# Order of the Nyquist row and of two weight splits in an attention, gated-MLP and Fourier kernel on one core

## The chip, the cores and the metric

The kernel runs on one NeuronCore of a Trainium2 chip. Its engines are called here as in the profile: PE (TensorE, matrix products; PEld is its weight load), DVE (VectorE), ACT (ScalarE), POOL (GpSimd) and SP (SyncE, which only issues DMAs). Each engine runs its own list of instructions in order, and engines wait for each other on semaphores. The metric is the device time of one execution in microseconds (us), and less is better. The time before is the median of three runs: 718.55, 721.84 and 721.86, so 721.84 us.

## The reference, cut to what matters

Three stages follow each other, for 4 batches (B) of 768 tokens (S) with 8 heads of 48 channels, 384 in all. The changes lie in the third stage and in the loading of its first weight.

```python
def _attn_ref(q, k, v, alpha):            # decayed linear attention
    for t in range(S):
        state = alpha[:, :, t, :, None] * state + np.einsum('bhd,bhe->bhde', k[:, :, t], v[:, :, t])
        y[:, :, t] = np.einsum('bhd,bhde->bhe', q[:, :, t], state)

def _moe_ref(x, w_in, g_ln, w_sg, b_sg, w_out):
    h = gelu_tanh(x @ w_in)
    u, v = (h[..., :d_ff // 2], h[..., d_ff // 2:])
    v_n = (v - mu) / np.sqrt(var + 1e-06) * g_ln
    v_s = np.einsum('ts,bsd->btd', w_sg, v_n) + b_sg[None, :, None]
    return x + (u * v_s) @ w_out

def _moe2_ref(x, w_ch1, w_ch2):
    X = np.fft.fft(np.fft.fft(x, axis=1), axis=2)
    u = x + np.real(X)
    un = (u - mu) / np.sqrt(var + 1e-06)
    return u + np.maximum(un @ w_ch1, 0.0) @ w_ch2
```

## The kernel before

*Numbers.* Large products run on float32r operands that are split into a hi part and a lo part; each product is three passes (hi x hi, hi x lo, lo x hi), `product`, L1178. Weights come from DRAM in pieces of 128 x 1536 (768 KB). Pieces 0 to 5 are `w_in`, `w_out`, `w_sg`; 6 to 8 are w_c1 (`w_ch1`; in rows `w_c`, or `w_c_0_117`, `w_c_1_118` for the first two); 9 to 11 are `w_c2`. A piece is split in one of two ways. The usual way: SP loads the raw piece into a stage, ACT copies it with a cast (hi, `split_hi`, L739), and DVE subtracts (lo = raw - hi, `split_lo`, L895). The other, for the pieces in `SUMMED` = (2, 3, 4): ACT writes -hi into the lo tile (`negative`, L744), and POOL issues a DMA that adds the raw piece from DRAM onto it (`sum_lo`, L693). `load_piece` decides when a stage is free: once the lo part of the piece before in the same stage is there, or, for a piece in `SUMMED`, its hi part. `wait_lo` is the consumer's wait.

*Stages of the work.* Phase 1 of batch b does the gated MLP of batch b and the attention of batch b + 1 beside it. Its steps stand in a table: "v" and "u" are the products with `w_in`, "s" 0 to 7 are the eight products with `w_sg`. After the product of s i PE does the `w_out` product of i - 1, which reads `gated_lo`. For every s DVE makes `gated` in two operations (L1025, L1029), ACT its hi part (L802), DVE its lo part (L971). In s 4 DVE also makes `x_half` (`add_x`, L979) from the banks that PE writes next. Phase 2 of batch b does the MLP with w_c1 ("h") and w_c2 ("o") and, beside it, the Fourier steps of batch b + 1. The Fourier steps of batch 0 stand beside phase 1 of the last batch, where there is no attention left to do (`LAST_P1_AT`). Phase 2 of batches 1 and 2 is one loop, run twice, on PE, ACT and DVE; phase 2 of batch 0 is code of its own. So the mixes of batch 0 run in the last phase 1, of batch 1 in phase 2 of batch 0, of batches 2 and 3 in the first and second pass of the loop. POOL and SP run without a loop.

*Fourier steps*, in the function `mixing` of each engine, in the order of `P2_AT`, `P2_FIRST_AT` and `LAST_P1_AT`:
- "fold", "folded": DVE adds mirrored quarters of the tokens (`x_quarters`; half of them are loaded by SP, the mirrored half by four indirect DMAs of POOL, L660), then hi and lo parts.
- "z": PE products with `seq_dft` into `FB[i % 3]` (FB are banks 5 to 7), and ACT copies them to `z` (L815).
- "nyquist": PE makes one row of output, the middle token (L1376, 2 instructions, 4 records of 97 columns), in columns 0 to 193 of `FB[1]`; ACT copies it (L818).
- "mix": PE makes all three tiles at once (L1388, 24 instructions, 48 records), tile i into `FB[TB[i]]`, `TB` = (2, 0, 1), so the third tile overwrites the row's bank and first waits for ACT's copy (`ahr_done`). ACT copies tile i (`even_odd`, L822), DVE makes sum and difference (L1072, L1073) and adds them to the residual rows (`u_new`, L1079, L1080), for i = 0 also the Nyquist row (L1086, L1087). The residual rows are loaded by `load_residual` on SP (L564, L567) and on POOL (three indirect DMAs, L660).
- "stats": DVE mean and variance; "norm", "turn", "turned": normalization, transposition, hi and lo parts of `ut`, the input of phase 2.

What sets the order: the tables at the top of the file, one for all engines, and each engine picks its part of a step. POOL's part of "mix" i is not run at "mix" in the last phase 1 but at "stats" i; in phase 2 it is run at "mix" i (`mixing` of POOL, L684 and L687, which waits for `mv2_done` of that tile's statistics). POOL issues the mirrored quarters of batch b + 2 where its list has "nyquist", ahead of its own part of that step.

SP's list at the place in question is: raw load of piece 6, raw load of piece 7 (same stage, so it waits for piece 6), the residual rows of batch 0, the store of x1, raw load of piece 8.

## Time and profile before

| what | value |
|---|---|
| time, median of three runs | 721.84 us |
| the three runs | 718.55, 721.84, 721.86 us |
| profiled execution: time, span | 720.12 us, 718.3 us |
| granted PE clock, mean | 0.995 |
| PE busy | 701.0 us, 98% |
| DVE busy | 451.8 us, 63% |
| ACT busy | 198.4 us, 28% |
| POOL busy | 80.0 us, 11% |

The span is the time from the first to the last instruction of the profiled execution. Busy time counts an engine's own operations; waits and DMA issues are not in it. PE busy is close to the whole span, and records of matmuls overlap each other, since they are pipelined.

### The profile page before, as it was taken

The page shows a single profiled execution, that of the slowest core. Times are in us where ns is not written, and L with a number is a line of the kernel's source. Part 1 is how long each engine was busy: PE and PEld are TensorE (multiplying, and loading weights), DVE is VectorE, ACT ScalarE, POOL GpSimd, SP SyncE. Part 2 cuts the span into 40 slices and gives each one's busy share as a digit, 9 for nine tenths or more (in the row PEclk, how much of TensorE's full clock was granted, in tenths as well). Part 3 has the DMA queues.
Part 4 walks back from the last instruction along what each step waited for, and adds up shares of the span by engine and source line. Part 5 has one row for each costly group of instructions (what it writes and reads, how often), then busy time and mean ns, then how long its engine had stood idle before and what let it go on. Part 6 is the DMA issues. An engine that isn't in the chain of part 4 may idle for free.

```text
span 718.3 us, 13452 instructions
## 1 busy us (share of the span) xinstructions
PE 701.0 (98%) x5578; PEld 670.6 (93%) x5578; DVE 451.8 (63%) x869; ACT 198.4 (28%) x369; POOL 80.0 (11%) x124
## 2 busy tenths in 40 slices
PE   7799989999999999999999999999999999999998
PEld 6689989889998999989999999999999999999998
DVE  7997868897768977668687747372543817331212
ACT  1438111242113411134415332232211422222111
POOL 1023000030001200042110512002210101000000
PEclk9999999999999999999999999999999999999999
DMA  9757132231332223061324403002110200000000
GB/s 295 208 139 182 52 100 84 83 97 55 91 93 71 63 54 97 35 212 44 112 77 165 144 20 92 1 34 67 53 59 1 76 23 33 0 34 1 5 29 34
DMA packets 21214, 55.90 MB, mean 78 GB/s; under 512 B 2388, under 2 KB 14808, under 8 KB 21160
## 3 DMA queue, kind: packets, MB, share of 16 engines
q1 hardware_dynamic: 18104, 44.53, 20.1%
q0 software_dynamic: 2912, 10.47, 5.6%
q8 instruction: 40, 0.66, 0.4%
q10 hardware_dynamic: 144, 0.13, 0.1%
q14 instruction: 14, 0.11, 0.1%
HBM read 45.66 MB, written 9.46 MB: 77 GB/s over the span
## 4 chain that ended last, share of the span: by engine, by line
PE 86%; DVE 10%; issue 2%; ACT 1%; DMA 1%; DVEq 0%; SPq 0%
PE bank L1178 74%; PE bank L1209 3%; PE bank L1241 2%; PE bank L1236 1%; PE bank L1273 1%; PE bank L1402 1%; PE bank L1388 1%; PE bank L1226 1%; DVE fwd L927 1%; DVE rev L915 1%; PE bank L1199 1%; DVE u_kept L1138 1%; DMA decay_k_q<-in_akq 1%; DVE sm L945 1%; DVE gated L1029 1%
## 5 line engine op out<-in xcount | busy, mean ns | idle before, releaser
L1178 PE MATMUL bank<-ut_hi,w_c 128*128 128x384 f32 x576 | 162.6, 338 | 0.0
L1125 DVE SCALAR_TENSOR_TENSOR hidden_lo<-bank,hidden_hi 128x384 fp32r<-128x384 f32 x96 | 53.3, 556 | 155.5 <-ACT hidden_hi L849 154.9
L1178 PEld LDWEIGHTS bank<-ut_hi,w_c 128*128 128x128 f32 x576 | 105.4, 188 | 0.4
L849 ACT ACTIVATE hidden_hi<-bank 128x384 fp32r<-128x384 f32 x96 | 47.2, 492 | 201.6 <-PE bank L1178 200.5
L1178 PE MATMUL bank<-w_c_hi,hidden_hi 128*128 128x384 f32 x288 | 96.6, 335 | 0.5 <-DVE u_kept L1138 0.5
L1178 PE MATMUL bank<-ut_lo,w_c 128*128 128x384 f32 x288 | 96.3, 334 | 0.0
L1178 PE MATMUL bank<-w_c_hi,hidden_lo 128*128 128x384 f32 x288 | 96.3, 334 | 0.0
L1178 PE MATMUL bank<-w_c_lo,hidden_hi 128*128 128x384 f32 x288 | 96.2, 334 | 0.0
L1178 PE MATMUL bank<-w_sg_hi,vn_hi 128*128 128x384 f32 x192 | 67.1, 350 | 0.0
L1178 PE MATMUL bank<-w_sg_lo,vn_hi 128*128 128x384 f32 x192 | 64.9, 338 | 0.0
L1178 PE MATMUL bank<-w_sg_hi,vn_lo 128*128 128x384 f32 x192 | 64.9, 338 | 0.0
L802 ACT CAST gated_hi<-gated 128x384 fp32r<-128x384 f32 x32 | 16.4, 513 | 152.2 <-DVE gated L1029 152.2
L1178 PEld LDWEIGHTS bank<-w_c_hi,hidden_hi 128*128 128x128 f32 x288 | 54.1, 188 | 1.5 <-issue 1.4
L1178 PEld LDWEIGHTS bank<-ut_lo,w_c 128*128 128x128 f32 x288 | 54.2, 188 | 0.0
L1178 PEld LDWEIGHTS bank<-w_c_lo,hidden_hi 128*128 128x128 f32 x288 | 54.1, 188 | 0.0
L1178 PEld LDWEIGHTS bank<-w_c_hi,hidden_lo 128*128 128x128 f32 x288 | 54.1, 188 | 0.0
L1178 PEld LDWEIGHTS bank<-w_sg_hi,vn_hi 128*128 128x128 f32 x192 | 36.5, 190 | 1.9
L1178 PEld LDWEIGHTS bank<-w_sg_hi,vn_lo 128*128 128x128 f32 x192 | 36.6, 191 | 0.0
L1178 PEld LDWEIGHTS bank<-w_sg_lo,vn_hi 128*128 128x128 f32 x192 | 36.5, 190 | 0.0
L1178 PE MATMUL bank<-w_out_hi,gated_hi 128*128 128x384 f32 x96 | 32.7, 340 | 2.0 <-DVE x_half L979 1.4
L1178 PE MATMUL bank<-x_hi,w_in_hi 128*128 128x384 f32 x96 | 32.9, 342 | 0.0
L945 DVE TENSOR_TENSOR sm<-bank,constants 128x512 f32<-128x512 f32 x42 | 27.0, 684 | 8.5 <-PE bank L1209 8.4
(193 smaller groups left out, 1339.8 us busy)
## 6 DMA issues: line engine op xcount, KB each, us to landing
decay_k_q<-in_akq SPq DMA_DIRECT2D x19, 673.8 KB, 5.0
x_scratch<-x_half SPq DMA_DIRECT2D x8, 579.0 KB
out_tiles<-u_kept SPq DMA_DIRECT2D x24, 192.0 KB, 2.0
values<-in_v SPq DMA_DIRECT2D x18, 192.0 KB, 5.0
x_quarters<-x_scratch SPq DMA_DIRECT2D x16, 168.9 KB
raw_first_a<-in_w_first SPq DMA_DIRECT2D x3, 768.0 KB, 10.2
raw_first_b<-in_w_first SPq DMA_DIRECT2D x3, 768.0 KB
raw_weights_b<-in_w_second SPq DMA_DIRECT2D x3, 768.0 KB
```

What stands on the lines that cost most here:

```text
L802: nc.scalar.copy(gs[0][:, i % 3, :], gt[:, i % 3, :]).then_inc(ghi_done, 1)
L849: nc.scalar.activation(hid[0][:, i % 4, :], HB[i % 2][:, 0:HS], ACT.Relu).then_inc(hhi_done, 1)
L915: nc.vector.tensor_tensor_scan(rev[:, NA - 2::-1], raw[:, NA - 1:0:-1], resets[:, NA - 1:0:-1], 1.0, ALU.mult, ALU.add).then_inc(rev_done, 1)
L927: nc.vector.tensor_tensor_scan(fwd[:], raw[:, 0:NA], resets[:], 0.0, ALU.mult, ALU.add).then_inc(fwd_done, 1)
L945: nc.vector.tensor_tensor(sm[:, :, x, :], sc[x][:].rearrange("p (a t) -> p a t", a=4), mask[:].unsqueeze(1).to_broadcast([P, 4, P]), ALU.m ...
L1029: nc.vector.tensor_tensor(gt[:, i % 3, :], gt[:, i % 3, :], ug[:, f, h * HS:(h + 1) * HS], ALU.mult).then_inc(gt_done, 1)
L1125: nc.vector.scalar_tensor_tensor(out=hid[1][:, i % 4, :], in0=HB[i % 2][:, 0:HS], scalar=0.0, in1=f32(hid[0][:, i % 4, :]), op0=ALU.max, o ...
L1138: nc.vector.tensor_tensor(ub[:, HT * i + j, :], ACC[j][:, 0:DM], ub[:, HT * i + j, :], ALU.add).then_inc(fin_done, 1)
L1178: ins = nc.tensor.matmul(dst, a, c, start=start and n == 0, stop=stop and n == len(passes) - 1)
L1199: ins = nc.tensor.transpose(ky[:, g * PR:(g + 1) * PR], kd[:, g, :], ident[0:PR, 0:PR])
L1209: ins = nc.tensor.matmul(sc[j][:, g * P:(g + 1) * P], kd[at, g, :], qu[at, g, :], start=True, stop=True)
L1241: ins = nc.tensor.matmul(ky[q, h * D:(h + 1) * D], sm[:, g, j, q], values[:, h * D:(h + 1) * D], start=c == 0, stop=True, skip_group_check ...
```

## The change

Four things are changed.

1. Table order: in `P2_AT`, `P2_FIRST_AT` and `LAST_P1_AT` the step "nyquist" follows "mix" 0, where it stood ahead of it.
2. The Nyquist row is no longer in columns 0 to 193 of `FB[1]` but in the free columns behind the mix tiles: its even half in `FB[0]`, its odd half in `FB[1]`, columns 388 to 484 of each. PE's wait for the row's copy in the middle of the mixes goes. ACT copies the row in two instructions; its copies of mix tiles 1 and 2 also wait for the row's product.
3. Pieces 6 and 7 (the first two of w_c1) join `SUMMED`: DVE's subtraction goes, ACT gets a negation each, and POOL a DMA each that adds onto SBUF. The stage that pieces 6, 7 and 8 share is then free once the hi part is made.
4. In `LAST_P1_AT` ACT's hi copy of piece 6 stands behind the four z steps, where it stood ahead of them, and that of piece 7 behind the second mix, where it stood ahead of the first. The negation follows each, and POOL's `sum_lo` stands at the same place.

```diff
-SUMMED = (2, 3, 4)
+SUMMED = (2, 3, 4, 6, 7)
...
-         10: [("nyquist", 0), ("mix", 0)], 11: [("stats", 0)], 12: [("mix", 1)], 13: [("stats", 1)], 14: [("mix", 2)], 15: [("stats", 2)],
+         10: [("mix", 0), ("nyquist", 0)], 11: [("stats", 0)], 12: [("mix", 1)], 13: [("stats", 1)], 14: [("mix", 2)], 15: [("stats", 2)],
...
-              ("s", 1): [("split", 6), ("z", 0), ("z", 1), ("z", 2), ("z", 3)],
-              ("s", 2): [("nyquist", 0), ("split", 7), ("mix", 0), ("stats", 0)],
-              ("s", 3): [("mix", 1), ("stats", 1)], ("s", 4): [("mix", 2)],
+              ("s", 1): [("z", 0), ("z", 1), ("z", 2), ("z", 3), ("split hi", 6), ("neg", 6)],
+              ("s", 2): [("mix", 0), ("nyquist", 0), ("stats", 0)],
+              ("s", 3): [("mix", 1), ("stats", 1), ("split hi", 7), ("neg", 7)], ("s", 4): [("mix", 2)],
...
+            def sum_lo(n):
+
+                pool.wait_ge(w_neg_done, SUMMED.index(n) + 1)
+                src, m = (w_first, n) if n < NP1 else (w_second, n - NP1)
+                pool.dma_start(pieces[n][1], src[:, m * PIECE:(m + 1) * PIECE],
+                               accum_op=ALU.add).then_inc(w_sum_in[n], 16)
...
+                            if what == "neg":
+                                sum_lo(n)
...
                 if step == "nyquist":
                     act.wait_ge(ny_done, m + 1)
-                    nc.scalar.copy(by_channel(fourier_tiles(m)[4][:]), by_parity(FB[1][0:1, 0:NL])).then_inc(ahr_done, 1)
+                    for odd in range(2):
+                        ins = nc.scalar.copy(by_channel(fourier_tiles(m)[4][:])[:, 0, odd], FB[odd][0:1, 2 * NL:2 * NL + KQ])
+                    ins.then_inc(ahr_done, 1)
                 if step == "mix":
                     act.wait_ge(mix_done, 2 * (KD * m + i + 1))
+                    if i > 0:
+                        act.wait_ge(ny_done, m + 1)
...
                 if step == "nyquist":
-                    pe.wait_ge(z_kept, 4 * m + 2)
                     for odd in range(2):
-                        ins = nc.tensor.matmul(FB[1][0:2, odd * KQ:(odd + 1) * KQ], zz[0:KQ - odd, 0, odd, HS:HS + 2],
+                        ins = nc.tensor.matmul(FB[odd][0:2, 2 * NL:2 * NL + KQ], zz[0:KQ - odd, 0, odd, HS:HS + 2],
                                                cs[0:KQ - odd, 0, odd, :], start=True, stop=True)
                     ins.then_inc(ny_done, 1)
                 if step == "mix" and i == 0:
                     pe.wait_ge(z_kept, 4 * (m + 1))
                     for i, e in itertools.product(range(HT), range(2)):
-                        if i == 2 and e == 0:
-                            pe.wait_ge(ahr_done, m + 1)
```

ACT's list in the last phase 1, before the change, from the `gated` of step s 1 to the second mix tile:

```order
L802 CAST gated_hi<-gated 128x384
L739 CAST w_c_0_117<-raw_weights_b 128x1536
L815 COPY z<-bank 97x2x194
L815 COPY z<-bank 96x2x194
L815 COPY z<-bank 97x2x194
L815 COPY z<-bank 96x2x194
L802 CAST gated_hi<-gated 128x384
L818 COPY nyquist_row_early<-bank 1x2x97
L739 CAST w_c_1_118<-raw_weights_b 128x1536
L822 COPY even_odd_early<-bank 128x2x2x97
L802 CAST gated_hi<-gated 128x384
L822 COPY even_odd_early<-bank 128x2x2x97
```

The same stretch of ACT's list after the change (`w_c_0_117<-w_c_0_117` is the negation):

```order
L807 CAST gated_hi<-gated 128x384
L820 COPY z<-bank 97x2x194
L820 COPY z<-bank 96x2x194
L820 COPY z<-bank 97x2x194
L820 COPY z<-bank 96x2x194
L744 CAST w_c_0_117<-raw_weights_b 128x1536
L749 ACTIVATE w_c_0_117<-w_c_0_117 128x1536
L807 CAST gated_hi<-gated 128x384
L831 COPY even_odd_early<-bank 128x2x2x97
L824 COPY nyquist_row_early<-bank 1x97 x2
L807 CAST gated_hi<-gated 128x384
L831 COPY even_odd_early<-bank 128x2x2x97
```

The hi copy of piece 6 has moved behind the z copies, with its negation. The hi copy of piece 7 has left this stretch; it comes right after its last row. SP's list has the same rows in the same order as before.

POOL's list from the x1 columns of the last phase 1 (`x_half`) to the second variance step of batch 1, before the change (`ve`, `rs` are the variance step):

```order
L651 COPY x_half<-x_half 128x3x2
L660 DMA x_quarters<-x_scratch,mirrored_rows 112x386 x4
L660 DMA u_new<-x_scratch,mirrored_rows 128x386 x3
L660 DMA x_quarters<-x_scratch,mirrored_rows 112x386 x4
L684 TENSOR_TENSOR ve_61<-mv_59,eps_c 128x2
L687 TENSOR_TENSOR rs_60<-ve_61,minus_half 128x2
L684 TENSOR_TENSOR ve_61<-mv_59,eps_c 128x2
L687 TENSOR_TENSOR rs_60<-ve_61,minus_half 128x2
```

The same stretch after the change:

```order
L658 COPY x_half<-x_half 128x3x2
L669 DMA x_quarters<-x_scratch,mirrored_rows 112x386 x4
L669 DMA u_new<-x_scratch,mirrored_rows 128x386 x3
L693 TENSOR_TENSOR ve_61<-mv_59,eps_c 128x2
L696 TENSOR_TENSOR rs_60<-ve_61,minus_half 128x2
L669 DMA x_quarters<-x_scratch,mirrored_rows 112x386 x4
L693 TENSOR_TENSOR ve_61<-mv_59,eps_c 128x2
L696 TENSOR_TENSOR rs_60<-ve_61,minus_half 128x2
```

The second group of four quarter loads (those of batch 2, beside the mixes of batch 1) has moved behind the first variance step. The same happens once more, a batch later.

## Rows read from the trace of the kernel before

**Rows 1.** The page: busy us (share) of PE to POOL; the chain by engine.
```profile
PE 701.0 (98%) x5578; PEld 670.6 (93%) x5578; DVE 451.8 (63%) x869; ACT 198.4 (28%) x369; POOL 80.0 (11%) x124
PE 86%; DVE 10%; issue 2%; ACT 1%; DMA 1%; DVEq 0%; SPq 0%
```

**Rows 2.** Waits of PE: who waited for whom, us in total, times, longest.
```profile
PE bank L1178 <- DVE x_half L979: 1.4, 1, 1.4
...
PE bank L1388 <- issue: 0.7, 2, 0.4
```

**Rows 3.** Timeline of PE, last phase 1: start, us, instruction, [idle before, releaser].
```profile
363.51 0.33 PE L1178 MATMUL bank<-w_out_hi,gated_hi 128*128 128x384 f32 x1
...
369.76 0.41 PE L1178 MATMUL bank<-w_out_hi,gated_hi 128*128 128x384 f32 x1 [1.41 <-DVE x_half L979]
```

**Rows 4.** Timeline of DVE, last phase 1.
```profile
351.53 0.62 DVE L1025 SCALAR_TENSOR_TENSOR gated<-bank,g_col,bias_sg 128x384 f32<-128x384 f32 x1 [3.88 <-PE bank L1178]
...
355.25 1.76 DVE L895 TENSOR_TENSOR w_c<-raw_weights_b,w_c 128x1536 fp32r<-128x1536 f32 x1 [1.37 <-ACT w_c L739]
...
357.68 0.56 DVE L1079 TENSOR_TENSOR u_new_early<-u_new_early,sum_diff_early 128x386 f32<-128x386 f32 x1
...
362.38 0.56 DVE L971 TENSOR_TENSOR gated_lo<-gated,gated_hi 128x384 fp32r<-128x384 f32 x1 [0.58 <-ACT gated_hi L802]
...
368.13 1.48 DVE L979 TENSOR_TENSOR x_half<-bank,y_by_token_odd 128x384 f32<-128x384 f32 x3
```

**Rows 5.** Timeline of PE at the mixes of batches 0, 1 and 3.
```profile
353.41 2.24 PE L1388 MATMUL bank<-chan_dft,z 97*64 97x97 f32 x48
...
430.48 1.98 PE L1388 MATMUL bank<-chan_dft,z 97*64 97x97 f32 x41
432.83 0.56 PE L1388 MATMUL bank<-chan_dft,z 96*64 96x97 f32 x7 [0.36 <-issue]
...
591.04 0.50 PE L1376 MATMUL bank<-chan_dft,z 97*2 97x97 f32 x4
591.47 2.24 PE L1388 MATMUL bank<-chan_dft,z 97*64 97x97 f32 x48
```

**Rows 6.** Timeline of ACT: last z copy, piece 7, first mix copies of batches 1, 3.
```profile
348.38 0.50 ACT L815 COPY z<-bank 96x388 f32<-96x388 f32 x1 [0.59 <-PE bank L1178]
...
353.75 1.46 ACT L739 CAST w_c<-raw_weights_b 128x1536 fp32r<-128x1536 f32 x1
...
432.94 0.51 ACT L822 COPY even_odd<-bank 128x388 f32<-128x388 f32 x1 [2.01 <-PE bank L1388]
...
592.44 0.52 ACT L822 COPY even_odd<-bank 128x388 f32<-128x388 f32 x1 [0.53 <-PE bank L1388]
```

**Rows 7.** Timeline of POOL beside the mixes of batch 1.
```profile
430.95 0.92 POOL L660 DMA_INDIRECT x_quarters<-x_scratch,mirrored_rows  x1 [0.30 <-issue]
437.82 0.18 POOL L684 TENSOR_TENSOR ve<-mv,eps_c 128x2 f32<-128x2 f32 x1 [5.94 <-DVE mv L1099]
...
443.90 0.22 POOL L684 TENSOR_TENSOR ve<-mv,eps_c 128x2 f32<-128x2 f32 x1 [5.10 <-DVE mv L1099]
```

**Rows 8.** Timeline of SP's DMA issues: piece 7 and the residual of batch 0.
```profile
347.67 0.36 SPq L515 DMA_DIRECT2D raw_weights_b<-in_w_second  x1
348.38 0.38 SPq L564 DMA_DIRECT2D u_new_early<-x_scratch  x1
```

**Rows 9.** DMA queues, 353 to 354 us, then 41 to 42: packets, MB, engines' share.
```profile
q0 software_dynamic: 124, 0.39, 101.7%
q1 hardware_dynamic: 5, 0.00, 1.3%
...
q0 software_dynamic: 33, 0.20, 98.9%
q1 hardware_dynamic: 2, 0.01, 3.1%
```

**Rows 10.** DMA issues by tile: KB each, median us from issue to landing.
```profile
w_out_lo<-in_w_first POOLq DMA_DIRECT2D x1, 768.0 KB, 8.0
```

More of the change, by code:

```diff
@@ L118 @@
                6: [("fold", 0)], 7: [("fold", 1)], 8: [("fold", 2), ("fold", 4)], 9: [("fold", 3), ("folded", 0)],
-               10: [("fold", 5), ("folded", 1), ("z", 0)], 11: [("z", 1), ("z", 2)], 12: [("z", 3)], 13: [("nyquist", 0), ("mix", 0)],
+               10: [("fold", 5), ("folded", 1), ("z", 0)], 11: [("z", 1), ("z", 2)], 12: [("z", 3)], 13: [("mix", 0), ("nyquist", 0)],
                14: [("stats", 0)], 15: [("mix", 1)], 16: [("stats", 1), ("mix", 2)], 17: [("stats", 2)],
@@ L688, in mixing @@
                                             ALU.pow).then_inc(rs2_done, 1)
-            def sum_lo(n):
-                pool.wait_ge(w_neg_done, SUMMED.index(n) + 1)
-                pool.dma_start(pieces[n][1], w_first[:, n * PIECE:(n + 1) * PIECE],
-                               accum_op=ALU.add).then_inc(w_sum_in[n], 16)
             for step, t in FIRST_POOL:
@@ L731, in beside_last_phase1 @@
                         split_hi(n)
+                    elif what == "neg":
+                        negative(n)
                     elif what in FOURIER_STEPS:
@@ L1422, in phase2 @@
                             pe.wait_ge(sb_done, 8 * B)
-                            wait_lo(pe, NP1 + KD - 2)
+                            for n in range(NP1, NP1 + KD - 1):
+                                wait_lo(pe, n)
                             product(HB[0][:, 0:HS], terms[:KD - 1], stop=False)
```

## The prediction

> **What bounds the kernel now.** I read the busy shares and the chain of waits first, then who waited on TensorE (PE), then the timelines around each of those waits, and last the DMA windows. PE is busy 98% of the span of 718.3 us and is 86% of the chain that ended last [rows 1]. So only two things can move the time: fewer PE instructions, or the few gaps in which PE stands. The change takes no matmul away (below), so the gaps are the whole prize. Within its reach are two kinds [rows 2]: one wait of 1.4 us for `x_half`, and "issue" gaps in front of mix matmuls, two times.
>
> The first [rows 3]: PE waits 1.41 us for VectorE's (DVE) `x_half` addition before it may start the `w_out` product at 369.76. The DVE timeline [rows 4] says why that is late. DVE idles 1.37 us until ScalarE (ACT) has made the hi copy of the second w_c1 piece, subtracts for 1.76 us from 355.25, and starts its first mix addition at 357.68; from there on work is queued one behind the other up to `x_half` at 368.13 to 369.61. Whatever DVE gains before 357.68 arrives at `x_half`, until PE's 1.41 us are used up.
>
> The second [rows 5]: a mix group has 48 matmul records. In batches 0 and 3 they run through in 2.24 us. In batch 1 there are 41, a hole, and 7 more, from 430.48 to 433.39: 2.91 us, so 0.67 us lost. Batch 2 reads the same, and the wait list counts two such gaps. ACT sees the first mix tile late too: its `even_odd` copy starts at 432.94, 2.46 us after the group's first record, against 592.44 - 591.47 = 0.97 us in batch 3 [rows 5, 6]. What batches 1 and 2 share, and 0 and 3 don't, is that GpSimd (POOL) is issuing the mirrored quarters of the following batch just then; in batch 1 its fourth indirect DMA runs from 430.95 to 431.87 [rows 7]. That is a coincidence of rows, not a proof.
>
> **The change part by part.**
>
> (a) Nyquist row behind the mixes. PE: four matmul records per batch stay four, now last instead of first. In batch 3 they take 591.47 - 591.04 = 0.43 us [rows 5], paid either way. The step from 384-column products to small ones is at one end of the group before and at the other now; nothing in the rows tells its cost apart, so I take 0, and as bounds a third of those 0.43 us in each of four places either way, 0.6 us. The wait for the row's copy in the middle of the mixes goes; in batch 3 the group ran through with it, so it held nobody: 0. ACT: one copy becomes two of 97 columns. The nearest row is the even_odd copy, 0.51 us for 388 columns [rows 6]; two copies cost at most 1.0 us and at least half of one, 0.25, in place of one that lies between. ACT is idle for 2 us before such steps [rows 6], so 0. DVE's row additions need these copies. The row is ready on PE some 2.7 us after the group's start (2.24 + 0.43) and copied by 3.5. DVE has the first tile at 0.97 + 0.51, and spends four operations, some 1.9 us, on it: 3.4. So 0.1 us on an engine that has slack there.
>
> (b) What moves with it on POOL. The order shows it: the four indirect `x_quarters` DMAs hang on the step "nyquist", POOL's variance step on "mix", and these two have changed places. POOL now waits for the statistics of the first mix, computes, and only then issues. In batch 1 the variance step starts at 437.82 [rows 7] and takes about 1 us, so the DMAs go out from 438.8 on, no longer at 427. They take 1.24 us each, to 443.8, and the next variance step stood at 443.90 in before [rows 7]: it fits with nothing to spare, and what comes after it (the normalization) waits for a third one anyway. The quarters are read by the folds of the next batch, tens of us later. Queued behind the waiting POOL instruction is nothing else. So the move costs 0, and the mixes of batches 1 and 2 lose their neighbour. I take the rows at their word: these mixes then look like batch 3's, -0.67 us twice, -1.34. Bounds: 0 (another cause) and -1.34.
>
> The Trainium skill, "Runtime: NRT & Kernel Launch", Instruction fetch mechanics, says that prefetch of instructions is sequential, in blocks, and that a taken branch breaks it. Batch 3 is the second pass of a loop whose first pass is batch 2, so a fetch stall would part them too, and (b) would bring nothing. Batch 0 is run for the first time as well and has no hole [rows 5], which speaks against it.
>
> (c) lo parts of the first two w_c1 pieces by accumulating DMA. DVE loses two subtractions of 1.76 us. The first lies before an idle time of 3.88 us [rows 4]: 0. The second stands in the queue above. With it gone, and ACT's hi copy (1.46 us from 353.75 [rows 6]) no longer ahead of the even_odd copy, that copy runs 0.97 us after the group's start, which is 353.41 - 0.43, so at 353.95, and DVE is through its two differences by 355.2: 2.5 us ahead of 357.68. ACT gains two negations; the nearest row is its hi copy of the same size, 1.46 us [rows 6]. The first pair (hi copy, negation) starts when the z copies end at 348.88 and ends at 351.8; the next thing ACT has to do comes with DVE's `gated` of 351.53 + 1.2 [rows 4]. The second pair lies behind the second mix copy, about 361.5 to 364.5; the `gated` of s4 is not there before 364.7. Cost 0, and one of 0.5 us if all comes early.
>
> But what is late next? DVE's first mix addition needs the residual rows, and the change delays their loading. On SP's queue the load of w_c1 piece 7 stands ahead of the residual. In before they went out at 347.67 and 348.38 [rows 8]. Now the hi copy of piece 6 stands behind four z copies (last ends 348.88 [rows 6]) and ends at 350.36, and only then does SP go on: 2.7 us later. In before SP's queue had moved all but 5 packets of both by 353 [rows 9]; 2.7 later is 355.7. POOL's three indirect residual loads, which keep their time, ran behind SP's in before (q0 with 101.7% of the engines' time from 353 to 354 [rows 9]) and now are ahead of them or between: they moved 0.6 MB at 0.39 MB in a us, 1.5 us. Of that 0 to 1.5 falls on SP's loads; I take 1.0. With 0.5 us until the semaphore is seen DVE starts at 357.2 instead of 357.68: -0.48 us. Lower end 356.2 (nothing ahead), the full -1.41. Upper end: the accumulating DMA of piece 6, issued at 352.5 behind POOL's indirects. One like it landed 8.0 us after its issue [rows 10], here 360.5; if it goes ahead, the residual is there at 361.3, +3.6 us. I take 357.2 since the engines serve first what came first: from 41 to 42 us an accumulating transfer on q0 has 98.9% of their time, and the SP load asked for 1.4 us after it 3.1% [rows 9].
>
> The Trainium skill, "DMA: Bandwidth & Descriptors", Queues, rings and completion order, says instead that an engine takes turns between queues packet by packet. By it the residual would share with the accumulating transfer from about 354 on and be there near 359, +1.3 us.
>
> Nobody waits for the two sums: the second is issued near 366 and lands near 374, and PE reads these pieces in phase 2, after 384. Their 1.5 MB may put off the load of piece 8 by 2 us; it has 11 us until ACT wants it.
>
> **Sum.** Against the profiled execution (span 718.3, whole time 720.12): -0.48 - 1.34 = -1.8, span 716.5. The three runs of before are 718.55, 721.84 and 721.86, so its profile lies between them. From the median: 721.84 - 1.8 = 720.0 us.
>
> **Rivals.**
> 1. *The residual comes late (slower).* Place: DVE before its first mix addition, waiting for SP's residual load. Every us beyond 357.68 arrives at PE, first in front of `w_out` of s3 (slack 363.51 - 362.94 = 0.57 us [rows 3, 4]), the rest at `x_half`. It decides from 359.0 on, where it has eaten the 1.34 us. With a landing at 360.2, between an even sharing and the upper end, it is +2.5 - 1.34 = +1.2: 723.0 us. For it: an accumulating transfer holds the engines fully at 0.20 MB in a us, half the rate of the others [rows 9]. Against: the residual is asked for 1.6 us before it.
> 2. *The holes at the mixes stay*, POOL's DMAs not being their cause: -0.5, so 721.4 us. For it: POOL's data also moves during batch 0's mixes (353 to 354 [rows 9]), and no hole comes. Against: the four batches split exactly as POOL's issuing does.
> 3. *Everything comes.* The residual is there by 356.3: -1.41 - 1.34 = -2.8, so 719.1 us. POOL's loads would have to be nearly through by 351; in before nothing of them had moved by then.
>
> **How the numbers follow.** Forecast 40%, rival 1 22%, rival 2 25%, rival 3 13%. A measurement of this kernel doesn't tell less than about 0.5% (3.6 us); its own runs lie 3.3 us apart. All cases lie within that, and only scatter or the far ends bring the time out of it. Faster by over 0.5% (below 718.2): half of rival 3 and a sixth of the forecast, 0.13. Slower (above 725.4): a third of rival 1, 0.07. Same: 0.80. Range 717.8 to 723.6: it takes in all four cases with some scatter, and leaves out the upper end of rival 1 and the lowest medians.
>
> **What the new profile would show.** Right: mixes of batches 1 and 2 without a hole, and `even_odd` about 1.0 us after their first record in all; POOL's quarters near 439; PE's wait for `x_half` near 0.9 us; DVE's wait before its first mix addition ended by a DMA, near 357. Wrong: holes of 0.7 us still there (rival 2); a wait of PE for `gated_lo` of s3, or a longer one for `x_half` (rival 1). A new gap on PE of over 1 us elsewhere, behind POOL's moved DMAs or at the start of phase 2, would break what I called hidden.

## The result: 723.35 us, slower than before by 0.36%

Timed side by side, the changed kernel takes 723.35 us (median of 22 runs, 718.99 to 726.37) and the kernel before 720.17 us (22 runs, 717.95 to 721.86). The ratio is 1.0036, with a 95% interval of 1.0022 to 1.0049: 1.6 to 3.5 us more. The forecast was 1.8 us less. The time lies inside the range and within the 0.5% called "same", but it moved to the other side: what happened is rival 1, at more than its price. That it lies inside the range is in part luck: the forecast started from 721.84 us, the median of three runs, and the median of 22 is 1.7 us lower. The loss of 3.2 us is larger than the 1.8 us that the range allowed above its start.

**The profile after.** The profiled execution has a span of 724.6 us and takes 726.37 us, the slowest of its 22 runs. It is 6.3 us longer than the profiled execution of before, and 2.5 us of that lie ahead of the changed place: the mixes of batch 0 begin at 355.45, where they began at 352.98. There PE's clock was low for longer after gaps near 101 to 103 us (granted 0.57 on average from 102 to 110, before 0.79). What follows is therefore read behind the start of these mixes. The page, as in [rows 1]:

```profile
PE 702.5 (97%) x5578; PEld 672.6 (93%) x5578; DVE 448.1 (62%) x867; ACT 201.8 (28%) x375; POOL 82.5 (11%) x126
PE 82%; DVE 10%; DMA 4%; issue 2%; ACT 1%; SPq 0%; DVEq 0%
```

PE has the same 5578 matmul records, and DMA has grown from 1% to 4% of the chain that ended last. PE's waits, against [rows 2] (us in total, times, longest):

```profile
PE bank L1187 <- DVE gated_lo L980: 4.6, 3, 4.1
```

The wait for `x_half` and the two gaps with "issue" in front of mix matmuls are gone from the list. In their place stands one wait of 4.1 us for `gated_lo`. PE's timeline around it, the counterpart of [rows 3, 5] (start, us, instruction, [idle before, releaser]):

```profile
355.45 2.24 PE L1394 MATMUL bank<-chan_dft,z 97*64 97x97 f32 x48
357.63 0.50 PE L1384 MATMUL bank<-chan_dft,z 97*2 97x97 f32 x4
...
365.79 0.34 PE L1187 MATMUL bank<-w_sg_hi,vn_lo 128*128 128x384 f32 x1
370.27 0.69 PE L1187 MATMUL bank<-w_out_hi,gated_hi 128*128 128x384 f32 x1 [4.14 <-DVE gated_lo L980]
370.75 0.52 PE L1187 MATMUL bank<-w_out_lo,gated_hi 128*128 128x384 f32 x1
371.07 0.52 PE L1187 MATMUL bank<-w_out_hi,gated_lo 128*128 128x384 f32 x1
...
375.77 0.33 PE L1187 MATMUL bank<-w_sg_hi,vn_lo 128*128 128x384 f32 x1
375.95 0.33 PE L1187 MATMUL bank<-w_sg_hi,vn_hi 128*128 128x384 f32 x1
...
437.69 2.24 PE L1394 MATMUL bank<-chan_dft,z 97*64 97x97 f32 x48
```

Two things are to be seen besides the gap. The mixes of batch 1 run through in 2.24 us, without the hole (those of batch 2 and 3 too, from 512.60 and 597.32). And behind the gap the starts of neighbouring matmuls lie 0.32 us apart until 375.5, and 0.17 or 0.18 from 375.77 on. The stretches say why (us; busy us and count of PE, PEld, DVE, ACT, POOL; granted clock of PE; DMA share, GB/s):

```profile
360.00:364.00 4.00, 4.00 (x25) 4.00 (x24) 0.00 (x0) 0.00 (x0) 0.00 (x0) 1.00 0.90 182
366.00:368.00 2.00, 0.13 (x1) 0.00 (x0) 1.89 (x8) 0.00 (x0) 0.00 (x0) 1.00 0.00 0
368.00:370.00 2.00, 0.00 (x0) 0.00 (x0) 1.39 (x3) 0.89 (x3) 0.91 (x2) 0.70 0.00 0
371.00:372.00 1.00, 1.00 (x4) 1.00 (x4) 0.96 (x3) 0.97 (x2) 0.00 (x0) 0.50 0.00 0
374.00:375.00 1.00, 1.00 (x5) 1.00 (x4) 0.42 (x2) 0.61 (x2) 1.00 (x2) 0.50 0.00 0
376.00:378.00 2.00, 2.00 (x13) 2.00 (x12) 1.87 (x5) 0.00 (x0) 0.24 (x1) 1.00 0.92 141
```

PE stood for 4.1 us, and the granted clock fell to 0.50 (1.2 of 2.4 GHz) in the gap and came back only near 375.6. So the gap costs twice: the 17 steps from 370.27 to 375.77 take 5.50 us, and at the full clock's 0.173 us each they would take 2.95, another 2.55 us.

The first line of that table holds the cause: from 360 to 364 DVE and ACT do nothing at all. DVE's timeline, against [rows 4]:

```profile
356.98 0.36 DVE L1081 TENSOR_TENSOR sum_diff_early<-even_odd_early 128x194 f32<-128x194 f32 x1 [0.63 <-ACT even_odd_early L831]
...
364.97 0.56 DVE L1088 TENSOR_TENSOR u_new_early<-u_new_early,sum_diff_early 128x386 f32<-128x386 f32 x1 [7.36 <-DMA x_middle_row_early<-x_scratch]
...
369.65 0.56 DVE L980 TENSOR_TENSOR gated_lo<-gated,gated_hi 128x384 fp32r<-128x384 f32 x1 [0.58 <-ACT gated_hi L807]
```

DVE has the difference of the first mix tile early, as meant, and then waits 7.36 us for the last of the residual rows, the 1.5 KB middle row. Counted from the first record of PE's mix group, the first mix addition starts at 364.97 - 355.45 = 9.52 us; before it was 357.68 - 352.98 = 4.70 [rows 4], and PE's row there is 0.43 us ahead of the mixes. SP issues that load here (against [rows 8]):

```profile
353.15 0.43 SPq L564 DMA_DIRECT2D u_new_early<-x_scratch  x1
353.62 0.39 SPq L567 DMA_DIRECT2D x_middle_row_early<-x_scratch  x1
```

and POOL its accumulating transfer of piece 6 another 1.1 us later:

```profile
353.76 0.95 POOL L669 DMA_INDIRECT u_new_early<-x_scratch,mirrored_rows  x1 [0.30 <-issue]
354.71 1.02 POOL L648 DMA_DIRECT2D w_c<-in_w_second  x1
```

The DMA queues in the windows 358 to 359, 359 to 360, 360 to 361 and 361 to 362 (packets, MB, share of 16 engines), q1 being SP's and q0 POOL's:

```profile
q1 hardware_dynamic: 144, 0.22, 70.7%
q0 software_dynamic: 23, 0.10, 39.2%
...
q0 software_dynamic: 53, 0.18, 88.0%
q1 hardware_dynamic: 54, 0.07, 22.0%
...
q0 software_dynamic: 33, 0.19, 98.0%
q1 hardware_dynamic: 8, 0.01, 2.8%
...
q0 software_dynamic: 35, 0.22, 105.4%
q1 hardware_dynamic: 3, 0.00, 1.5%
```

The trace's records of single packets show three steps. Ahead of the residual on SP's own queue is the raw load of piece 7, 128 packets of 6144 bytes that begin from 353.80 to 357.98. The residual and the middle row are 385 packets of 1536 bytes from 356.74 on, and 370 of them have begun by 360. The accumulating transfer, issued at 354.71 behind POOL's own residual loads, begins its first packet at 359.30, so it meets only the tail. The last 15 packets come in at 1 to 5 in a us (the 8 of q1 above hold three of 4 bytes), with 1 to 3% of the engines, while the accumulating transfer has 96 to 105% from 360 to 363. The tail has two strings of packets. One is at 361.11, 361.64, 362.17 and 362.70. This is the end of the other, each packet of which takes 0.079 us:

```
start us   362.22   362.76   363.29   363.82   364.36
```

They are 0.53 us apart. The packets of q0 (6144 bytes) take 0.479 us each (median of its 128). The records don't name the DMA engine, but the spacing fits one small packet behind each big slow one on the two engines that still have rows to move. The last lands at 364.43, and DVE starts 0.54 us later.

**Where the time went.** From the first record of a mix group to that of the next batch's, before and after: batch 0 to 1 77.08 and 82.24 us, +5.16; batch 1 to 2 75.60 and 74.91, -0.69; batch 2 to 3 85.38 and 84.72, -0.66. The first is 4.14 for the gap, 2.55 for the clock and -1.41 for the `x_half` wait that is gone, 5.3 in all. The sum is +3.8; the medians say +3.2. The seven runs with a mean granted clock of 0.990 or 0.991 have a median of 724.3 us, the seven with 0.995 one of 721.8. That fits runs that lose less to the clock at this gap, but it isn't shown: only the profiled run has a clock by place, and part of its low clock lies near 103 us.

### The profile page after: what moved, and what is told of

Read it like the earlier page. It is cut to its first block, busy times and chain, and to the rows that moved or that the text cites. A ratio compares the mean times of both kernels' runs of the same rounds, so it can differ in the third digit from the quotient of the medians.

```text
span 724.6 us, 13457 instructions
## 1 busy us (share of the span) xinstructions
PE 702.5 (97%) x5578; PEld 672.6 (93%) x5578; DVE 448.1 (62%) x867; ACT 201.8 (28%) x375; POOL 82.5 (11%) x126
## 3 DMA queue, kind: packets, MB, share of 16 engines
HBM read 47.23 MB, written 9.46 MB: 78 GB/s over the span
## 4 chain that ended last, share of the span: by engine, by line
PE 82%; DVE 10%; DMA 4%; issue 2%; ACT 1%; SPq 0%; DVEq 0%
PE bank L1187 72%; PE bank L1218 3%; PE bank L1250 2%; DMA x_middle_row_early<-x_scratch 2%; PE bank L1245 1%; DMA w_sg_lo<-in_w_first 1%; DMA decay_k_q_b<-in_akq 1%; DVE rev L924 1%; PE bank L1408 1%; PE bank L1282 1%; PE bank L1394 1%; DVE fwd L936 1%; PE bank L1208 1%; PE bank L1235 1%; DVE u_kept L1147 1%
```

## The experiments

Each ratio is against the kernel before, timed on the same chip beside it. The twelve profiled executions differ by up to 3.5 us already ahead of the changed place (batch 0's mixes begin between 351.91 and 355.45 us), so I read each trace also by a stretch: from the first record of batch 0's mix group to the end of the span. "Start" is when DVE begins its first mix addition, counted from that same record.

| kernel | median, us | before, us | ratio (95%) | stretch, us | start, us |
|---|---|---|---|---|---|
| before | | 720.17 | | 365.3 | 4.70 |
| after | 723.35 | 720.17 | 1.0036 (1.0022 to 1.0049) | 369.15 | 9.52 |
| nyq_only | 718.1 | 720.95 | 0.9956 (0.9942 to 0.997) | 363.9 | 4.14 |
| sums_only | 725.2 | 720.95 | 1.0058 (1.004 to 1.0076) | 369.95 | 9.46 |
| residual_first | 719.03 | 720.95 | 0.9975 (0.9964 to 0.9987) | 363.5 | 4.24 |
| sum_late | 719.8 | 720.95 | 0.9984 (0.9973 to 0.9995) | 364.0 | 4.72 |
| plain_six (one run) | 721.67 | 719.35 | | 367.2 | 6.41 |
| pool_moved | 718.96 | 719.35 | 0.9996 (0.9981 to 1.0012) | 363.9 | |
| pool_back | 722.04 | 719.35 | 1.0056 (1.0032 to 1.008) | 368.3 | 9.01 |
| seven_only | 717.73 | 719.35 | 0.9973 (0.9958 to 0.9987) | 363.0 | 2.29 |
| nyq_again | 718.49 | 719.74 | 0.9984 (0.9971 to 0.9997) | 363.4 | 4.14 |
| seven_again | 718.35 | 719.74 | 0.9978 (0.9964 to 0.9993) | 362.8 | 2.36 |

### The two halves of the change: nyq_only, sums_only

nyq_only has the Nyquist row behind the mixes and what moves with it on POOL, and leaves the weights as before:

```diff
-SUMMED = (2, 3, 4, 6, 7)
+SUMMED = (2, 3, 4)
-              ("s", 1): [("z", 0), ("z", 1), ("z", 2), ("z", 3), ("split hi", 6), ("neg", 6)],
-              ("s", 2): [("mix", 0), ("nyquist", 0), ("stats", 0)],
-              ("s", 3): [("mix", 1), ("stats", 1), ("split hi", 7), ("neg", 7)], ("s", 4): [("mix", 2)],
+              ("s", 1): [("split", 6), ("z", 0), ("z", 1), ("z", 2), ("z", 3)],
+              ("s", 2): [("split", 7), ("mix", 0), ("nyquist", 0), ("stats", 0)],
+              ("s", 3): [("mix", 1), ("stats", 1)], ("s", 4): [("mix", 2)],
```

> The Nyquist part alone (row behind the mixes, free columns, POOL's quarters behind the first variance step); weights split as before. Theory (the two parts add up, and the loss sits in the weights part): no hole in any of the four mix groups, PE wait for x_half stays near 1.4 us, time 1.3 us below before (ratio 0.998). Rival (the loss comes from the Nyquist part, from POOL's moved DMAs): a new gap in phase 2 or slower than before.

sums_only is the other half: the weights of after, with the row's old banks, waits and order in all tables. In the last phase 1:

```diff
-              ("s", 2): [("mix", 0), ("nyquist", 0), ("stats", 0)],
+              ("s", 2): [("nyquist", 0), ("mix", 0), ("stats", 0)],
```

> The accumulating transfers for pieces 6 and 7 alone, Nyquist row and its order as before. Theory: DVE waits some 7 us for the residual, PE waits 4 us for gated_lo and then has the clock at 0.5 for 5 us, and the two holes of 0.67 us at the mixes stay: 5.2 us above before (ratio 1.007), the slowest of the four. Rival (noise or the Nyquist part makes the loss): within 1 us of before.

Measured: one half is faster than before, the other slower, by its stretch and its median ratio by more than the whole change, though the two intervals overlap. PE of sums_only, then of nyq_only:

```profile
367.81 0.44 PE L1183 MATMUL bank<-w_out_hi,gated_hi 128*128 128x384 f32 x1 [4.07 <-DVE gated_lo L976]
...
435.28 2.06 PE L1393 MATMUL bank<-chan_dft,z 97*64 97x97 f32 x42
437.64 0.55 PE L1393 MATMUL bank<-chan_dft,z 96*64 96x97 f32 x6 [0.30 <-issue]
```
```profile
430.69 2.24 PE L1394 MATMUL bank<-chan_dft,z 97*64 97x97 f32 x48
```

sums_only has the 4.1 us gap and keeps the holes at the mixes of batches 1 and 2. In nyq_only all mixes run through (`x48` in 2.24 us), and PE's wait for `x_half` is 0.86 us. So the loss is the weights' and the gain the Nyquist half's: by the stretch +4.6 and -1.4. These don't add up to the +3.85 of after exactly (+3.2). The clock is a part of that. Behind its gap of 4.07 us sums_only had the full clock again from 372 on, 4.2 us after PE resumed, and lost 1.7 us by the starts of its matmuls; after had it 5.4 us after PE resumed and lost 2.55. So gaps of nearly the same length didn't cost the same.

### What makes the residual late: residual_first, sum_late, plain_six

residual_first is after with two lines of SP's list exchanged:

```diff
-            load_piece(sp, NP1 + 1)
             load_residual(0)
+            load_piece(sp, NP1 + 1)
```

> The changed kernel with SP's residual load ahead of the raw load of piece 7. Theory A (the loss is the delay on SP's queue, which puts the residual's tail beside the accumulating transfer): the residual lands before 356 us on before's scale, DVE does not wait for it, PE has no wait for x_half: 2.7 us below before (ratio 0.996). Theory B (the accumulating transfer would slow the residual wherever it stands): DVE still waits some us and the time is at or above before.

sum_late is after with POOL's accumulating transfer of piece 6 put behind the first tile's statistics, so that it can't run beside the residual's loads:

```diff
-                            if what == "neg":
+                            if (what, n) == ("neg", 7):
                                 sum_lo(n)
                             if what == "stats":
                                 mixing(0, "mix", n)
+                                if n == 0:
+                                    sum_lo(6)
```

> The changed kernel with POOL's accumulating DMA of piece 6 behind the first statistics step instead of right behind the residual loads; SP's queue stays as in the changed kernel. Theory A (the delay on SP's queue alone makes the loss): DVE's wait stays several us, as long as in the changed kernel. Theory B (the accumulating transfer beside the residual makes it): DVE starts its first mix addition near my forecast's time, some 4 us after the first record of the mix group, PE's gap shrinks below 1.4 us, and the time is 1.8 us below before (ratio 0.9975).

plain_six is after with piece 6's transfer on POOL as a plain copy of the same bytes at the same place; it leaves out the addition.

```diff
-                pool.dma_start(pieces[n][1], src[:, m * PIECE:(m + 1) * PIECE],
-                               accum_op=ALU.add).then_inc(w_sum_in[n], 16)
+                if n == 6:
+                    pool.dma_start(pieces[n][1], src[:, m * PIECE:(m + 1) * PIECE].bitcast(F32R)).then_inc(w_sum_in[n], 16)
+                else:
+                    pool.dma_start(pieces[n][1], src[:, m * PIECE:(m + 1) * PIECE],
+                                   accum_op=ALU.add).then_inc(w_sum_in[n], 16)
```

> The changed kernel with POOL's DMA of piece 6 as a plain copy of the same bytes to the same tile at the same place in its queue: it leaves out the addition, so the lo part of piece 6 is the raw piece. Theory C (the accumulation makes the transfer hold the engines twice as long, and with that it starves SP's queue): DVE's first mix addition comes near 5 us after the first record of the mix group, against 9.5 in the changed kernel, and PE's gap is under 1 us. Rival (any 768 KB on POOL's queue there does it): DVE's wait is within 1 us of the changed kernel's 7.4.

DVE's first mix addition in residual_first, in sum_late and in plain_six:

```profile
358.03 0.56 DVE L1088 TENSOR_TENSOR u_new_early<-u_new_early,sum_diff_early 128x386 f32<-128x386 f32 x1 [2.09 <-DMA u_new_early<-x_scratch,mirrored_rows]
```
```profile
358.94 0.56 DVE L1090 TENSOR_TENSOR u_new_early<-u_new_early,sum_diff_early 128x386 f32<-128x386 f32 x1 [2.57 <-DMA x_middle_row_early<-x_scratch]
```
```profile
359.10 0.56 DVE L1091 TENSOR_TENSOR u_new_early<-u_new_early,sum_diff_early 128x386 f32<-128x386 f32 x1 [4.26 <-DMA x_middle_row_early<-x_scratch]
```

Either remedy alone takes the loss away; both kernels are faster than before. In residual_first SP's rows have landed at 352.58, 1.2 us ahead of the mix group, and they are no longer the last: DVE now waits 2.09 us for POOL's mirrored rows, a wait I had not listed. Those rows share the engines with the raw load of piece 7 from 352.5 on, and from 355.8 on with the accumulating transfer behind them. PE still waits 0.96 us for `x_half`, so this kernel falls short of the 2.7 us expected of it. In sum_late SP's issue is as late as in after (2.31 us ahead of the mix group, there 2.30, before 4.60), and no accumulating transfer is in its way. The last row lands 4.29 us after the group's first record, and the addition starts at 4.72, the same as before. PE's wait for `x_half` is still 1.45 us. So the later issue eats the gain and no more. With a plain transfer beside it the start is 6.41, with the accumulating one 9.52: 1.7 us for sharing the engines at all, and 3.1 us more with the slow packets. These are single traces; other kernels with the accumulating transfer in this place have 9.46 (sums_only) and 9.01 (pool_back). In plain_six the last small packets of one string of q1 are 0.30 to 0.33 us apart (357.08, 357.38, 357.68, 357.99, 358.31), beside q0's packets of 0.26 us (median of 128): the same taking of turns, at a shorter beat. The queue of the plain transfer from 357 to 358:

```profile
q0 software_dynamic: 67, 0.39, 104.0%
```

PE's gaps there are 1.04 us for `gated_lo` and 1.81 us for `x_half`.

### What made the holes at the mixes: pool_moved, pool_back

pool_moved is the kernel before with only POOL's quarter loads put behind the variance step:

```diff
-                    if (step, i) == ("nyquist", 0) and b + 2 < B:
-                        load_quarters(b + 2)
                     mixing(b + 1, step, i)
+                    if (step, i) == ("mix", 0) and b + 2 < B:
+                        load_quarters(b + 2)
```

> The kernel before with one thing changed: POOL issues the quarters of the following batch behind its first variance step, as in the changed kernel; the Nyquist row stays ahead of the mixes, with PE's wait for its copy in their middle. Theory P (POOL's DMAs beside the mixes make the holes): no hole in batches 1 and 2, 1.3 us below before (ratio 0.998). Rival Q (PE's wait for the row's copy inside the group makes them): both holes of 0.67 us stay, time as before.

pool_back is after with these loads at their old time, ahead of the variance step:

```diff
-                    if (step, i) == ("nyquist", 0) and b + 2 < B:
+                    if (step, i) == ("mix", 0) and b + 2 < B:
```

> The changed kernel with one thing undone: POOL issues the quarters of the following batch ahead of its first variance step, beside the mixes, as before. Theory P: holes of about 0.7 us are back in batches 1 and 2 and the time is 1.3 us above the changed kernel's (ratio to before near 1.006). Rival Q: no holes, the time as the changed kernel's (1.0036).

PE of pool_moved at batch 1, then POOL and PE of pool_back:

```profile
430.52 2.24 PE L1388 MATMUL bank<-chan_dft,z 97*64 97x97 f32 x48
```
```profile
433.01 0.93 POOL L669 DMA_INDIRECT x_quarters<-x_scratch,mirrored_rows  x1 [0.30 <-issue]
434.24 0.93 POOL L669 DMA_INDIRECT x_quarters<-x_scratch,mirrored_rows  x1 [0.30 <-issue]
```
```profile
433.34 2.24 PE L1394 MATMUL bank<-chan_dft,z 97*64 97x97 f32 x48
```

ACT beside the same groups: the row's copy in before, then the first mix copy in pool_moved and in pool_back:

```profile
430.59 0.34 ACT L818 COPY nyquist_row<-bank 1x194 f32<-1x194 f32 x1 [1.50 <-issue]
```
```profile
431.49 0.52 ACT L822 COPY even_odd<-bank 128x388 f32<-128x388 f32 x1 [0.53 <-PE bank L1388]
```
```profile
434.31 0.54 ACT L831 COPY even_odd<-bank 128x388 f32<-128x388 f32 x1 [1.93 <-PE bank L1394]
```

Moving POOL's loads alone closes the holes, and its stretch is 1.4 us shorter, the forecast's 1.34. But in pool_back they are issued right beside the mixes, and, against what I expected, there is no hole either. ACT's first mix copy follows the group's first mix record by 0.97 us in both, where with a hole it took 2.46 [rows 5, 6]. So POOL's loads are one condition of a hole and not its whole cause: the other is something of the old group, its order or the wait for the row's copy in its middle, or the timing, since POOL's last load begins 0.47 us after the first mix record in before and 0.90 us after it in pool_back. The wait alone didn't hold PE: in before the copy that it is for ended at 430.93, and the hole opens at 432.46, 41 records in, where the third tile begins with the 33rd. Moving POOL's loads and the new place of the row each remove the holes alone, and the gain is had once. The medians of pool_moved, 0.4 us apart, don't show the 1.4 us; the interval (-1.4 to +0.9 us) just touches it. A kernel meant to part the order of the row from the wait in the middle (row_first_free: the row ahead of the mixes in the free columns, without the wait) gave no time, so how the conditions work together stays open.

### The version without the loss: seven_only, nyq_again, seven_again

Piece 6 is split in the usual way, ahead of the z steps; only piece 7 is by the accumulating transfer, late in phase 1.

```diff
-SUMMED = (2, 3, 4, 6, 7)
+SUMMED = (2, 3, 4, 7)
-              ("s", 1): [("z", 0), ("z", 1), ("z", 2), ("z", 3), ("split hi", 6), ("neg", 6)],
+              ("s", 1): [("split", 6), ("z", 0), ("z", 1), ("z", 2), ("z", 3)],
```

> The changed kernel with piece 6 split in the usual way ahead of the z copies and only piece 7 by the accumulating DMA, so that SP goes on as early as in before and no accumulating transfer runs beside the residual. Theory: DVE does not wait for the residual and is 1.8 us ahead at the first mix addition, PE waits neither for x_half nor for gated_lo for more than 0.3 us; 2.8 us below before (ratio 0.996) and at or below the kernel with the Nyquist part alone. Rival (accumulating transfers in this stretch cost wherever they are, by the x1 store and the load of piece 8 behind them): at or above the Nyquist part alone (0.9956) by over 1 us.

Both seven_only and nyq_only had come out faster than before, but not side by side, so the two were timed again beside each other, on another chip.

> The Nyquist part alone once more, beside the version with piece 7 alone: by the traces from the start of batch 0's mixes to the end it took 363.9 us, before 365.3, so 1.4 us below before (ratio 0.998). If the 3.2 us measured earlier are real and not scatter of the first 350 us, the ratio comes at 0.9956 again.

> Piece 7 alone by the accumulating DMA, with the Nyquist part, on the same chip as the Nyquist part alone: by the traces 363.0 against 363.9 us from batch 0's mixes on, so 0.9 us faster than the Nyquist part alone (ratio to before 0.9968 against 0.998). If the accumulating transfer of piece 7 cost as much as it frees, the two would be equal within 0.2 us in that stretch.

Side by side they are 0.14 us apart in the median, which these runs can't tell from nothing. Each is faster than before by an interval that leaves out 1, and after was slower than before. The 0.9 us that I expected between them isn't shown, nor were the 2.8 us below before expected of seven_only (1.6 measured, 2.3 by the stretch). nyq_only's first ratio of 0.9956 (5 runs, another chip) did not come again: its second is 0.9984. The two traces still differ by what the weights' half was meant to bring. DVE of nyq_again, then of seven_again:

```profile
355.04 1.76 DVE L904 TENSOR_TENSOR w_c<-raw_weights_b,w_c 128x1536 fp32r<-128x1536 f32 x1 [0.81 <-ACT w_c L744]
...
357.47 0.56 DVE L1088 TENSOR_TENSOR u_new_early<-u_new_early,sum_diff_early 128x386 f32<-128x386 f32 x1
```
```profile
356.89 0.56 DVE L1088 TENSOR_TENSOR u_new_early<-u_new_early,sum_diff_early 128x386 f32<-128x386 f32 x1 [0.21 <-DMA u_new_early<-x_scratch,mirrored_rows]
```

The subtraction is gone, the addition starts 1.8 us sooner after the group's start (2.36 against 4.14), and the wait of PE for `x_half`, 0.8 us in nyq_again's list, doesn't occur in seven_again's. The stretches are 363.4 and 362.8.

## Why the prediction was wrong

**The failed step** is the residual's term of part (c): "I take 357.2 since the engines serve first what came first". It was worth -0.48 us in the sum. Measured, the addition started 4.8 us later than before, counted from the group's start, and the term with all that hangs on it came to +5.2 us. The forecast had all rows landed at 356.7, which is 3.7 us after the group's start. In sum_late, without the accumulating transfer beside them, they landed at 4.3; in after at 9.0. So the delay of SP's issue and POOL's own loads were sized 0.6 us too low, which is what the -0.48 us hung on, and the accumulating transfer, which the forecast put at nothing, is the other 4.7. The 0.5 us from landing to DVE's start was right (0.54). Three pieces make up the difference.

1. *The order of service.* The rows I rested on [rows 9] show an accumulating transfer with 98.9% of the engines and a later load with 3.1%. I read this as "the first has the engines". It shows as well what becomes of any load beside such a transfer, first or not: two small packets got in. In after the load was asked for 1.1 us earlier than the transfer, got its bulk through by 360, and its tail was slowed to one packet per 0.53 us. The Trainium skill, "DMA: Bandwidth & Descriptors", Queues, rings and completion order, has the rule: every engine goes round the queues that have work for it, a packet at a time. The trace agrees on the turns, with 0.53 us between small packets beside big ones of 0.479. It differs on their size: the page gives a packet typically 9 to 17 descriptors, and here single records of 1536 bytes took turns with single records of 6144. My estimate by that rule, +1.3 us, was too low since it shared the time evenly between queues; packets of 1536 and 6144 bytes, at 0.079 and 0.479 us, share it 1 to 6.
2. *The upper end was too low.* Even with all in its way I had the addition at 361.3, 8.3 us after the group's start. It came at 9.52.
3. *The clock.* No term stood for what a gap of PE does to PE's clock. In the trace of before the longest gap at this place was 1.41 us [rows 3], and no loss behind it was to be seen. Behind 4.14 us it was 2.55 us more. Elsewhere in the trace of before the clock did fall behind a shorter gap: PE waited 1.53 us ahead of 101.79 and was busy 0.47 of the 2 us from 100 to 102, and the granted clock averages 0.52 from 103 to 106.

**Rival 1 is what happened**, by its mechanism and at its place: PE waits first for `gated_lo` of s 3. Its price, +1.2 us, was for a landing 7.2 us after the group's start and without the clock. The gap itself follows from its own rule: 4.82 us later, less the slack of 0.57, is 4.25; it was 4.14.

**The sign that I named held**: "a wait of PE for `gated_lo` of s3 (rival 1)".

**The holes (part b)**: -1.34 forecast, -0.69 and -0.66 measured. The size and the remedy were right, and pool_moved shows that the move is enough. The reason is only half right: I took what parts batches 1 and 2 from 0 and 3 for the cause, and pool_back shows that a second condition is needed. Against it I had set the rule on fetching instructions (the Trainium skill, "Runtime: NRT & Kernel Launch", Instruction fetch mechanics), which ties a stall to a taken branch. The trace doesn't bear it out: the loop's jump back lies ahead of batch 3, which has no hole, and pool_moved, whose PE list is that of before, has none in batch 2 either.

**POOL's move at no cost**: right in effect. The loads go out from 445.78 on, behind the variance step:

```profile
444.61 0.19 POOL L693 TENSOR_TENSOR ve<-mv,eps_c 128x2 f32<-128x2 f32 x1 [30.69 <-DVE mv L1108]
...
445.78 0.99 POOL L669 DMA_INDIRECT x_quarters<-x_scratch,mirrored_rows  x1 [0.18 <-issue]
...
450.87 0.21 POOL L693 TENSOR_TENSOR ve<-mv,eps_c 128x2 f32<-128x2 f32 x1
```

As figured, they fit with nothing to spare: POOL's next variance step follows without a wait, where DVE had let it wait 5.10 us before [rows 7]. PE has no new gap behind it.

**The Nyquist row (part a)**: 0 forecast. Its four records still end 0.5 us after they begin, and the group as a whole is as long; nothing waits for the row's copies. nyq_only even starts the addition 0.56 us sooner (4.14 against 4.70), since piece 7's hi copy no longer waits behind the row's copy on ACT: a gain that came with the order of the steps and that I had not seen. PE's wait for `x_half` fell from 1.41 to 0.86 us by it.

**ACT's negations and the late sums**: hidden, as said. ACT's first pair ends at 354.24, before DVE's `gated` needs it:

```profile
352.75 1.49 ACT L749 ACTIVATE w_c<-w_c 128x1536 fp32r<-128x1536 f32 x1
355.24 0.51 ACT L807 CAST gated_hi<-gated 128x384 fp32r<-128x384 f32 x1 [1.00 <-DVE gated L1038]
```

The chances gave the side that came 22% as rival 1, and the forecast 40%. From the same rows rival 1 had earned more: the rows showed what an accumulating transfer does to its neighbour, and for "first come, first served" there was one row that read both ways.

## What to carry to other kernels

Before a bulk transfer is put beside a small load that an engine waits for, look at the packets: here the last small packets came in one per big packet of the other queue, so a tail that isn't through when the bulk transfer's data begins is late by its number of packets on that engine times the big packet's duration, though the load was issued first. Put the awaited load ahead of every other load on its own queue, or the bulk transfer behind it; each cured it here. And when a change can open a gap of several us on a matmul engine that is otherwise full, price the clock with it, as a range: two gaps of 4.1 us cost 1.7 and 2.55 us here.

## What the runs showed of the hardware

- An accumulating transfer from DRAM into SBUF moves 0.19 to 0.22 MB in a us with all engines busy, since its 6144-byte packets take 0.479 us each; a plain copy of the same bytes took 0.26 us a packet in plain_six, 0.39 MB in a us at 104% of the engines. So beside an accumulating transfer the engines read as full (101% and more from 360 to 362 in after) at about half the throughput.
- The granted clock falls also within a gap of about 4 us (0.70 as the mean from 368 to 370), is 0.50 on return and full again 5.4 us after PE resumed. In sums_only, after 4.07 us, PE went on at 0.33 to 0.34 us a matmul at first, and the means then read 0.62 (368 to 370) and 0.53 (370 to 372). In before no such fall followed the gap of 1.41 us at this place (1.00 from 368 to 372). In plain_six, two gaps of 1.04 and 1.81 us some 5 us apart were followed by a fall as well:

```profile
364.00:372.00 8.00, 5.79 (x32) 5.50 (x33) 7.04 (x19) 3.95 (x5) 2.06 (x4) 1.00 0.25 35
372.00:374.00 2.00, 2.00 (x9) 2.00 (x8) 1.91 (x4) 0.00 (x0) 0.00 (x0) 0.55 1.05 215
```

- A hole of about 0.7 us opened in a group of 48 small matmuls only where POOL was issuing indirect DMAs and the group was of the old form (batches 1 and 2 of before and of sums_only); neither alone was enough (pool_moved, pool_back). The cause isn't known.
